# q's softmax statistics through scratch memory to a feature-major q, instead of turning q on TensorE

## What is computed

```python
q_s = q - np.max(q, axis=-1, keepdims=True)
q_s = np.exp(q_s)
q_s = q_s / (np.sum(q_s, axis=-1, keepdims=True) + 1e-09)
...
kv = np.einsum('bhsd,bhse->bhde', k_s, v)
return np.einsum('bhsd,bhde->bhse', q_s, kv).astype(np.float32)
...
h = x @ w_in
...
v_s = np.einsum('ts,bsd->btd', w_sg, v_n) + b_sg[None, :, None]
gated = u * v_s
return (x + gated @ w_out).astype(np.float32)
```

## Time and profile before

| what | us |
|---|---|
| median of 3 runs | 932.77 (932.71 to 933.64) |
| time of the profiled execution | 931.71 |
| its span in the trace | 929.8 |

### The profile page before, as it was taken

How to read it: one execution, slowest core, us unless ns; L and a number is a source line. 1 busy time by engine, 2 the same in 40 slices (tenths; PEclk the granted TensorE clock), 3 DMA queues, 4 the chain that set the end, 5 groups by cost and what they waited for, 6 DMA issues and landing times.

```text
span 929.8 us, 14721 instructions
## 1 busy us (share of the span) xinstructions
PE 914.8 (98%) x5972; PEld 856.0 (92%) x5972; DVE 609.1 (66%) x958; ACT 380.6 (41%) x579; POOL 356.5 (38%) x232
## 2 busy tenths in 40 slices
PE   6999999999999999999999999999999999999998
PEld 4899999998998999999999999998999999999987
DVE  7788948656666577475464797866766656757650
ACT  7652624425334245244144354534343333434331
POOL 6684736436454464263205133322222313222320
PEclk9999999999999999999999999999999999999999
DMA  8817244061261340511331302020202020200001
GB/s 292 244 61 233 76 131 130 20 202 52 52 196 38 96 166 12 159 52 30 120 119 30 125 1 74 12 86 23 74 24 74 23 85 23 74 24 24 23 25 54
DMA packets 51202, 78.10 MB, mean 84 GB/s; under 512 B 4416, under 2 KB 23104, under 8 KB 50240
## 3 DMA queue, kind: packets, MB, share of 16 engines
q1 hardware_dynamic: 46528, 67.74, 23.2%
q10 hardware_dynamic: 4608, 9.44, 2.7%
HBM read 57.23 MB, written 18.89 MB: 82 GB/s over the span
## 4 chain that ended last, share of the span: by engine, by line
PE 89%; DVE 4%; POOL 2%; issue 2%; ACT 1%; DMA 1%; SPq 0%; POOLq 0%; ACTq 0%; DVEq 0%
PE psum L468 53%; PE psum L460 29%; PE psum L545 3%; PE psum L630 2%; PE psum L529 1%; PE psum L580 1%; DVE plain_arena L1346 1%; POOL plain_arena L1692 1%; DVE plain_arena L1377 1%; DMA plain_arena<-in_q_first 1%; POOL plain_arena L1680 1%; DMA split_arena<-split_arena 0%; PE psum L506 0%; DVE split_arena L1447 0%; DVE plain_arena L1224 0%
## 5 line engine op out<-in xcount | busy, mean ns | idle before, releaser
L468 PE MATMUL psum<-split_arena 128*128 128x288 f32 x4032 | 556.8, 296 | 1.0 <-DVE split_arena L1332 0.5
L468 PEld LDWEIGHTS psum<-split_arena 128*128 128x128 f32 x4032 | 544.1, 189 | 6.7 <-issue 1.1
L460 PE MATMUL psum<-split_arena 128*128 128x512 f32 x1248 | 295.8, 391 | 0.1
L460 PEld LDWEIGHTS psum<-split_arena 128*128 128x128 f32 x1248 | 230.4, 188 | 46.4 <-DVE plain_arena L1423 0.6
L1815 POOL TENSOR_TENSOR plain_arena<-plain_arena 128x576 f32<-128x576 f32 x64 | 107.7, 1683 | 277.9 <-ACT plain_arena L992 277.9
L1468 DVE SCALAR_TENSOR_TENSOR plain_arena<-plain_arena 128x576 f32<-128x576 f32 x64 | 96.2, 1503 | 2.3
L1463 DVE TENSOR_SCALAR plain_arena<-plain_arena 128x576 f32<-128x576 f32 x64 | 36.0, 563 | 87.2 <-ACT plain_arena L986 87.2
L1735 POOL TENSOR_TENSOR plain_arena<-plain_arena 128x576 f32<-128x576 f32 x32 | 46.5, 1453 | 108.6 <-DVE plain_arena L1402 108.6
L986 ACT ACTIVATE plain_arena<-psum 128x576 f32<-128x576 f32 x64 | 41.6, 650 | 105.0 <-PE psum L468 73.9
L992 ACT ACTIVATE plain_arena<-plain_arena 128x576 f32<-128x576 f32 x64 | 43.7, 683 | 42.9 <-DVE split_arena L1632 39.8
L1632 DVE TENSOR_TENSOR split_arena<-plain_arena,split_arena 128x576 fp32r<-128x576 f32 x64 | 53.2, 832 | 10.6 <-ACT split_arena L998 9.7
(11 more groups left out here) (95 smaller groups left out, 805.1 us busy)
## 6 DMA issues: line engine op xcount, KB each, us to landing
x_dram<-plain_arena ACTq DMA_DIRECT2D x32, 288.0 KB, 2.1
plain_arena<-x_dram SPq DMA_DIRECT2D x8, 1152.0 KB, 5.8
out_rows<-plain_arena SPq DMA_DIRECT2D x36, 256.0 KB, 2.0
plain_arena<-in_kT SPq DMA_DIRECT2D x7, 1152.0 KB, 9.0
plain_arena<-in_q SPq DMA_DIRECT2D x7, 1024.0 KB, 5.9
plain_arena<-in_k SPq DMA_DIRECT2D x7, 1024.0 KB, 5.7
plain_arena<-in_v SPq DMA_DIRECT2D x28, 256.0 KB, 3.2
plain_arena<-in_w_out SPq DMA_DIRECT2D x6, 512.0 KB, 4.5
```

Source lines behind the costliest of these rows:

```text
L460: mm = e.matmul(out, stat[s], mov[m], start=first and n == 0, stop=last and n == 2, skip_group_check=True)
L468: mm = e.matmul(out[:, h, 0:NH], stat[s], mov[m][:, h * NH:(h + 1) * NH], start=first and n == 0, stop=last and n == 2, skip_group_check=True)
```

## The change

From batch 2 on q is loaded twice. `q_heads` is a copy laid out flat, 36 rows of 64 features on each of 128 partitions (`q_flat`), and serves the statistics alone. Its maxima and inverse sums are stored to scratch memory (`store_q_max`, `store_q_rec`), and read back broadcast over the 64 partitions of a head (`spread_q_max`, `spread_q_rec`) into the high half of `qT`, which serves as landing place. `qT_rows` is q feature-major (`q_rows`, in the same place in SBUF as `k_view`). On it POOL subtracts the maxima (`sub_q_rows`), ACT exponentiates a second time (`exp_q_rows`), POOL multiplies by the inverse sums (`scale_q_rows`), ACT and DVE split (`hi_q_rows`, `lo_q_rows`), in four blocks of 128x576. TensorE turns q for batch 1 alone, in body 0.

```diff
+        TPP = D * T // (P * HD)
+        assert T % TPP == 0 and TPP % 2 == 0
+        q_flat = plain(0, TPP, HD)
+        q_rows = plain(KT_AT, DT, T)
...
+        q_max_dram = nc.dram_tensor("q_max_dram", [B, P * TPP], F32, kind="Internal").ap()
+        q_rec_dram = nc.dram_tensor("q_rec_dram", [B, P * TPP], F32, kind="Internal").ap()
...
-                if b == 1:
-                    e.wait_ge(q0_turned, DT)
-                else:
-                    e.wait_ge(q_turned, (b - 1) * NJ)
+                if b > 1:
+                    if b == 2:
+                        e.wait_ge(q_turned, NJ)
+                    else:
+                        e.wait_ge(q_rec, q_parts(b))
+                    e.dma_start(q_flat, q_heads[b].rearrange("p (t c) -> p t c", c=HD)).then_inc(q_in, 16)
+                    return
+                e.wait_ge(q0_turned, DT)
...
-                if isinstance(b, int) and b == 2:
+                if b == 2:
                     e.wait_ge(w_out_lo, len(W_OUT))
+                elif b > 3:
+                    e.wait_ge(q_lo, q_lows(b - 1))
                 e.dma_start(k_view, kT[b].rearrange("(p a) s -> p a s", a=DT)).then_inc(kT_in, 16)
...
+            def store_q_max(b):
+
+                e.wait_ge(q_max, q_parts(b + 1))
+                e.dma_start(q_max_dram[b].rearrange("(p t) -> p t", t=TPP), qmax[:, 0:TPP]).then_inc(q_max_out, 16)
...
+            def store_q_rec(b):
+
+                e.wait_ge(q_rec, q_parts(b + 1))
+                e.dma_start(q_rec_dram[b].rearrange("(p t) -> p t", t=TPP), qrec[:, 0:TPP]).then_inc(q_rec_out, 16)
...
+            def spread(stat, ds, arrived):
+
+                for h in HALVES:
+                    e.dma_start(f32(qT[0][h * HD:(h + 1) * HD, ds, :]),
+                                stat.rearrange("(d h t) -> h d t", d=DT, h=2)[h, ds, :].partition_broadcast(HD)
+                                ).then_inc(arrived, 16)
...
+            def spread_q_max(b):
+
+                e.wait_ge(x_done, b * DT)
+                e.wait_ge(q_max_out, 16 * (b - 1))
+                spread(q_max_dram[b], slice(0, DT), q_max_in)
+
+            def spread_q_rec(b, i):
+
+                e.wait_ge(q_rows_sub, DT * (b - 2) + 2 * i + 2)
+                if i == 0:
+                    e.wait_ge(q_rec_out, 16 * (b - 1))
+                spread(q_rec_dram[b], slice(2 * i, 2 * i + 2), q_rec_in[i])
+
+            def load_q_rows(b):
+
+                e.wait_ge(k_neg, negs(min(b + 1, B - 1)))
+                e.dma_start(q_rows, qT_rows[b].rearrange("(d p) t -> p d t", p=P)).then_inc(q_rows_in, 16)
...
                     if n is not None:
                         load_kT(n)
+                    store_q_max(m + 1)
+                    store_q_rec(m + 1)
+                    if n is not None:
+                        load_q(n)
+                    spread_q_max(m + 1)
                     load_v(m + 1, 2)
+                    load_q_rows(m + 1)
+                    if n is not None:
+                        spread_kmax(n)
+                    load_v(m + 1, 3)
                     move_tail(m)
-                    load_v(m + 1, 3)
+                    spread_q_rec(m + 1, 0)
+                    spread_q_rec(m + 1, 1)
                 if n is not None:
-                    if not (isinstance(m, int) and m == 0):
-                        spread_kmax(n)
                     load_v(n, 0)
                     load_v(n, 1)
-                    load_q(n)
+                    if m == 0:
+                        load_q(n)
                     load_k(n)
-                    if isinstance(m, int) and m == 0:
+                    if m == 0:
                         spread_kmax(n)
                     load_v(n, NJ - 1)
...
-            e.wait_ge(q_turned, (B - 1) * NJ)
-            e.wait_ge(k_neg, negs(B - 1))
+            e.wait_ge(q_lo, q_lows(B))
...
-                    e.wait_ge(q_lo, b * NJ)
+                    e.wait_ge(x_lo, b * DT)
                 else:
                     e.wait_ge(x_lo, b * DT + d)
+                e.wait_ge(q_lo, NJ if b == 1 else q_lows(b) + d + 1)
...
-                    for d in range(DT - 1):
+                    for d in range(DT):
                         v_part(m, 0, [d])
                         v_part(m, 1, [d])
                         if d + 2 < DT:
                             x_piece(m, d + 2)
-                    if a is not None and not late:
-                        turn_q(a, 0)
-                    v_part(m, 0, [DT - 1])
-                    v_part(m, 1, [DT - 1])
-                if late:
-                    turn_q(a, 0)
 
                 v_part(m, 2, list(range(DT)))
                 for f in range(FT):
                     u_unit(m, f)
-                    if f % 2 == 0 and not start:
-                        kv_and_turn(f // 2)
+                    if f % 2 == 0 and not start and a is not None:
+                        kv_piece(a, f // 2)
...
-                    elif f < 2:
-                        kv_and_turn(2 + f)
-                    elif f == 2 and a is not None:
-                        kv_piece(a, NJ - 1)
+                    elif f < 3 and a is not None:
+                        kv_piece(a, 2 + f)
...
+                if b > 1:
+                    at = slice(u * TPP // 2, (u + 1) * TPP // 2)
+                    e.wait_ge(q_sub, q_parts(b) + u + 1)
+                    e.activation(q_flat[:, at, :], q_flat[:, at, :], ACT.Exp).then_inc(q_exp, 1)
+                    return
...
+            def exp_q_rows(b, d):
+                e.wait_ge(q_rows_sub, DT * (b - 2) + d + 1)
+                e.activation(q_rows[:, d, :], q_rows[:, d, :], ACT.Exp).then_inc(q_rows_exp, 1)
+
+            def hi_q_rows(b, d):
+                e.wait_ge(q_rows_norm, DT * (b - 2) + d + 1)
+                e.activation(qT[0][:, d, :], q_rows[:, d, :], ACT.Identity).then_inc(q_hi, 1)
...
                     gelu_u(m, 0)
-                else:
-                    tile(0)
...
-                    if f % 2 == 0 and not start:
-                        tile(f // 2 + 1)
...
+                elif a is not None:
+                    for d in range(DT):
+                        exp_q_rows(a, d)
...
-                    elif f < 2:
-                        tile(3 + f)
+                    elif a is not None and f in (1, 2):
+                        hi_q_rows(a, 2 * f - 2)
+                        hi_q_rows(a, 2 * f - 1)
...
+                if b > 1:
+                    at = slice(u * TPP // 2, (u + 1) * TPP // 2)
+                    e.wait_ge(q_in, 32 + 16 * (b - 1))
+                    if b > 2:
+                        e.wait_ge(q_max_out, 16 * (b - 2))
+                    e.tensor_reduce(qmax[:, at], q_flat[:, at, :], X, ALU.max).then_inc(q_max, 1)
+                    return
...
+            def lo_q_rows(b, d):
+                e.wait_ge(q_hi, q_lows(b) + d + 1)
+                e.tensor_tensor(qT[1][:, d, :], q_rows[:, d, :], f32(qT[0][:, d, :]), ALU.subtract).then_inc(q_lo, 1)
...
-                    tile(0)
...
-                    for f in range(0, FT, 2):
-                        tile(f // 2 + 1)
-                        if n is not None:
-                            max_k(n, f // 2)
+                    if n is not None:
+                        max_k(n, 0)
+                        max_k(n, 1)
                     if a is None:
                         lo_w2(3)
                     for f in range(FT):
                         if f > 0:
                             lo_g(m, f - 1)
                         affine(m, f)
-                        if f < 2:
-                            tile(3 + f)
+                        if f in (1, 2) and a is not None:
+                            lo_q_rows(a, 2 * f - 2)
+                            lo_q_rows(a, 2 * f - 1)
...
+            def sub_q_rows(b, d):
+                if d == 0:
+                    e.wait_ge(q_max_in, 32 * (b - 1))
+                    e.wait_ge(q_rows_in, 16 * (b - 1))
+                e.tensor_tensor(q_rows[:, d, :], q_rows[:, d, :], f32(qT[0][:, d, :]),
+                                ALU.subtract).then_inc(q_rows_sub, 1)
+
+            def scale_q_rows(b, d):
+                e.wait_ge(q_rows_exp, DT * (b - 2) + d + 1)
+                e.wait_ge(q_rec_in[d // 2], 32 * (b - 1))
+                e.tensor_tensor(q_rows[:, d, :], q_rows[:, d, :], f32(qT[0][:, d, :]),
+                                ALU.mult).then_inc(q_rows_norm, 1)
...
-                if a is not None and not start:
-                    for u in range(NU):
-                        scale_q(a, u)
...
+                    if a is not None:
+                        for d in range(DT):
+                            sub_q_rows(a, d)
                 for f in range(FT):
                     gate(m, f)
+                    if not start and a is not None and f < 2:
+                        scale_q_rows(a, 2 * f)
+                        scale_q_rows(a, 2 * f + 1)
...
+        "q_heads": inputs["q"].reshape(B, 128, -1),
```

(1 more changed line is left out.)

58 lines of the change are left out of this document (37 added, 21 removed).

## The result

| | us | runs |
|---|---|---|
| after, median | 963.05 (962.01 to 964.23) | 4 |
| before, beside it | 932.96 (932.71 to 933.64) | 4 |
| ratio | 1.032, 95% interval 1.030 to 1.034 | |
| profiled execution after | 963.46, span 961.6 | |

The account below looks back on a forecast made before the run. TensorE's own instructions were taken to bound each body; five bodies with 6.9 us wait plus 2.3 slow clock minus 1.78 transposes, and body 6's 1.78 gain, gave +35.3 us, a median of 968, range 938 to 985.

Parts of the forecast that it names:

- The transposes: TensorE, bodies 1 to 6: five turn_q a body at 0.35 us go, 1.78 a body, 10.7 us in all.
- TensorE's arrival: Body 3, first L630: TensorE comes to its wait for move_tail at 249.2 instead of 250.28, with three turns less ahead.
- The second `max_k`: DVE, body 3: the second max_k of batch 5 begins at 242.1 and ends at 243.4.
- The store behind `q_rows`: SP's queue, body 3: store of k's maxima, issued at 244.0, waits behind q_rows' 1152 KB and returns at 250.2.
- The copy: SP, body 3: move_tail, issued at 251.2 behind broadcast and load of v, lands at 256.1; TensorE waits 6.9 us.
- The clock: TensorE behind each wait, bodies 1 to 5: clock falls, 5 us slow at 47%, 2.3 us a body, bounds 0 and 4.0.
- rival 1: TensorE, bodies 1 to 5: wait comes but clock does not fall or rises at once; +23.8, 956.6; chance 0.14.
- q's chain: POOL, ACT and DVE work on q_rows: third lo_g at about 271, TensorE near 273; no second wait, 2 us margin.
- Rival 3: POOL's list: copy in time, but subtractions hold the gate; 3.0 - 1.78 = 1.2 a body, 937; chance 0.13 with another rival.
- Body 6: No round trip of k's maxima, so no wait: 1.78 us gained, body length about 61.4 us.
- The new transfers: DMA, each body: stores, broadcasts and second load of q, some 4 MB; bandwidth is there, places in the queue matter.
- The sum: Whole kernel: 5 x (6.9 + 2.3 - 1.78) - 1.78 = +35.3 on the profiled 931.71, so 967.0, median 968.

Follow-up runs that it names:

- The filled wait: Kernel after, with 36 matmuls of 128x288 whose result nothing reads put ahead of TensorE's wait for the copy in bodies 1 to 5: 955.58 us, ratio 1.023.
- the last run: Kernel after with SP, POOL, ACT and DVE lists reordered; its last edit holds third-stage weight loads until batch 6's stores of x land: 923.92 us, ratio 0.990.
- two of the steps on the way (974 and 960 us): Kernel after with SP's copy and load of v ahead of q_rows: 974.07 us; that plus POOL, ACT and DVE lists reordered: 960.4 us.

## Why the prediction was right, and where its sizes were off

The sign, the mechanism and the place were right, and 963.05 lies in the range; 968 was 5 us too high.

- **The transposes**, 10.7 predicted: too little. Body 6, in which TensorE waits 0.29 us only, is 2.0 us shorter, not 1.78, so six bodies give about 12 us. The reading took the 0.35 us from the start of a turn to what follows; it missed that the turn itself begins 0.89 us behind the `kv_piece` ahead of it (242.56 to 243.46 in the kernel before), where without a turn the next work begins after 0.81 (248.68 to 249.49 after). The run with one transpose of four can't show this part.
- **TensorE's arrival** at the copy, 249.2 in the times of before: 263.4 - 14.32 = 249.1. The second `max_k`, 243.4: its end at 257.57 is 243.25. Right, and with them the reading that one `turn_q` less ahead of `sum_tail` moves DVE by 1.6 us.
- **The store behind `q_rows`**, 6.2 us from issue to return: 5.33. `q_rows`, issued at 257.59, landed after 5.5 us, at 263.1, and the store was back at 263.36: it doesn't pass the 1152 KB on its queue. By itself it takes 1.44 to 1.46 in two experiments, less than the 2.66 that I read from the earlier trace rows, where it stood behind a copy and a load. Here the first half of the rule in the Trainium skill (DMA: Bandwidth & Descriptors, Queues, rings and completion order), the engines take the descriptors of one ring in order, is what the runs show; nothing of its second half, that a later write may finish earlier, is seen.
- **The copy**, landed at 256.1: 269.23 - 14.32 = 254.9. The miss of 1.2 is the store's: issued 0.3 earlier than I had it and back 0.9 sooner. The copy itself took 4.87 from its issue, where I had 4.9. So the wait was 5.88 in body 3; in the mean it was 6.5 against 6.9, and 32.3 against 34.5 in all.
- **The clock**, 2.3 a body: it fell, as predicted, against rival 1, and cost about 1.9. I took 5 us of slow work behind each wait, from the kernel's start; measured are 2.9 to 6.0, in the mean 4.0, since a part of each slow stretch lay in the wait. The filled wait agrees with this.
- **q's chain**, hidden with 2 us of margin: in the kernel after TensorE waits 0.3 us for it in all, in body 6. In bodies 1 to 5 it was hidden by the wait for the copy and by nothing else. With the copy in time it costs 3.5 us a body, so this is the weakest step of the prediction: there was no margin in the lists, only in the wait. Rival 3 priced it at 3.0 - 1.78 with durations read where POOL ran without DVE beside it, and without the clock.
- **Body 6**, 61.4: 61.11. The new transfers make 3.5 MB a body, not "some 4"; nothing hangs on it.
- **The sum** of the measured terms is 32.3 + 9.4 - 12.1 = +29.6, of 30.1. Against the prediction's +35.3, 2.2 of the miss are the waits, 2.1 the clock and 1.4 the transposes. The two profiled runs differ by more, 31.8, of which 1.6 stand at the kernel's start (last section), which no term had.

The run with only SP's order changed shows the cause by itself: +31.5 us without any of the new transfers. What the new transfers add is that the store stands behind `q_rows` (5.33 us instead of 1.44). The order isn't forced by the change either: the last run keeps every new transfer and instruction.

## What to carry to other kernels

Before a transfer is put into a queue, ask what stands behind it that someone waits for: here 31.5 us hang on a 128 KB copy that is ready early and stands behind a row that waits for something else. The repair can make the same fault with another row, as the copy ahead of `q_rows` did. A first wait hides a second: once the copy was in time, POOL's list cost 3.5 us a body, and then came the meeting of a load with the stores of x; each came to light only when the one ahead was taken away, and two of the steps on the way (974 and 960 us) looked like dead ends. When a wait is shortened but not removed, the clock's share of the loss can grow: 10.8 us less of waiting were 7.3 us less of time.

## What the runs showed that I had not expected

- **DVE and POOL slow each other** when both read their operands from SBUF. A `lo_q_rows` takes 0.74 us with POOL idle, 1.98 beside a scaling and 2.67 beside a `sub_q`; a `gate` takes 1.95 instead of 1.42, a `sub_q` 2.6 instead of 2.1. In the stretch of 7.17 us DVE's three at 0.74 and POOL's two at 2.1 would make 6.4 one after the other, and the first of the three met the last scaling besides. `affine`, which reads one operand from PSUM, keeps its 0.81 beside POOL. The Trainium skill (SBUF — State Buffer, SBUF: two separate sides) says that a DVE operation with two SBUF inputs and a GpSimd operation that reads SBUF take a shared port in turns, each for its whole length; these rows agree. No run here puts it to the test by itself.
- **A shorter wait can have more slow work behind it**: 20.1 us of work at the low level behind 32.3 us of waits, 25.8 behind 21.5.
- **The start differs from run to run by 1.6 us**: in the profiled run after, ten matmuls that begin at 14.67 still take 2.18 us, where the same ten took 1.35 in the earlier trace rows, and body 0 comes to the tail of its `v_part` at 39.37 instead of 37.76. The profiled run with only SP's order changed has its clock at the low level from 13.0 to 16.4, and the run before has not. TensorE does the same work in the first 20 us of all three, so the change isn't a likely cause, but no run shows what is.
